# Both parts of a head's phi stacked in 128 rows for the product with the memory matrix

## The chip, the cores and the metric

The kernel runs as one program on one core of a Trainium2 chip. The metric is the device time of one execution in microseconds (us); lower is better.

## The reference

Four batches of eight heads (32 heads, 16 pairs of neighbouring heads), 576 tokens and 64 channels a head. Each head gets causal softmax attention and a second term, a read from a memory matrix; the two are mixed by a gate. Two MLP layers follow.

```python
scores = scale * q @ k.T                      # causal, then softmax -> a
local = a @ v
q_p = phi(q)                                  # phi(x) = where(x > 0, x, exp(x) - 1) + 1
mem_ret = einsum('bhsd,bhde->bhse', q_p, M_prev)          # M_prev: 64 x 64 for each head
mem_norm = einsum('bhsd,bhd->bhs', q_p, z_prev)[..., None] + 1e-06
mem_out = mem_ret / mem_norm
g = sigmoid(beta)
attn = g * mem_out + (1 - g) * local
x = attn as (B*S, H*D)
x = (sigmoid(x @ w_gate) * (x @ w_val)) @ w_out           # 2304 tokens, 512 -> 1536 -> 512
h = x @ w_in                                              # 512 -> 2048
out = (h * clip(h + 3, 0, 6) / 6) @ w_out2                # 2048 -> 512
```

## The kernel before

**Precision.** TensorE multiplies numbers rounded to fp32r. The kernel splits an operand x into a rounded part `hi` and a remainder `lo = x - hi` and adds several products. ScalarE (ACT) writes `hi` as it copies a block out of PSUM, VectorE (DVE) then writes `lo` with a subtraction that reads the same PSUM block and `hi`.

**The product with the memory matrix.** phi of a pair lies with tokens in the partitions; TensorE turns it (`turn_phi`, L859), so that a PSUM block has channels in the partitions: rows 0 to 63 belong to the even head of the pair, rows 64 to 127 to the odd one. Before, `move_hi` (L1140) rounds the block into `phit_hi` (128 rows, 576 columns) and `move_lo` (L1488) writes `phit_lo`. Each comes in two pieces: piece 0 has 512 columns and lies in bank TURN, piece 1 has 64 columns and shares a bank with a turned block of probabilities. The weights `m_hl[odd]` (128 x 128) hold head `odd`'s matrix in its own 64 rows alone, rounded in its own 64 columns, the remainder in the other 64; the rest of the tile is zero (a memset on GpSimd, L715). `times_mem` runs four matmuls a head: 128 columns with `phit_hi`, 128 with `phit_lo`, 448 with `phit_hi`, 448 with `phit_lo`, into `head_out` in banks AOUT and AOUT + 1. `times_v` adds the probabilities times v to the same place. Then ACT copies the 64 rows with the remainders' products to `x_low` (`x_lower`, L1198) and DVE adds them to the other 64 rows, into `x_new` (`x_sum`, L1544), which frees the banks (`x_done`).

**The order of work.** Each engine runs an instruction stream in a fixed order; semaphores tie the streams together. The first pairs (0 to 3) are prepared in a lead-in (`lead`) with fp32 data and don't use `m_hl`. Pairs 4 to 15 do. Pair 4's phi is turned and moved in the last step of the lead-in, that of pairs 5 to 15 in the steps of the main part. The main part is a sequence of steps `step(n, p, ...)`, with p = 0 and p = 1; two of them make a pair. In each, TensorE does, slot by slot (i = 0 to 4): scores of head (n, p), units of the first MLP (`FILL`: G and V are gate and value units, O output units), the products of the head of pair n - 1 (`times_mem`, `times_v`, in slot 0), and transposes of the probabilities of the head before (`turn_head`, L846). All products of the kernel have line L805 in the profile, since one helper `mm` issues them.

In a step with p = 1 slot 0 ends with `turn_phi(n, 0)`, which waits for `phi_ready`: DVE scales phi (`phi_scaled`, L1522) after the value unit V5 of the same slot. Slot 1 then begins with the scores and the output units O0 and O1, and ends with `turn_head(.., 0)`, which writes into bank AOUT + 1 and so waits for `x_done`. In the same slot ACT's order is: phi piece 0, the exponential of tile 1, `x_lower`, the rounding of the memory matrix (`high_m`, L1205), two weight blocks. DVE's is: phi piece 0, `x_sum`, two results Y (L1705 or L1707), and `low_q` (L1456), which writes the remainder of the next head's q from two SBUF tiles. The mask of the next score tile (L1540) is behind it; `scores` for tile i + 2 waits for the mask of tile i.

```python
elif i < 2:
    pe.wait_ge(x_done, 2 * n + odd)              # in turn_head
if j == 0:
    pe.wait_ge(phi_ready, n + 1)                 # in turn_phi
```

GpSimd splits k and v and writes the remainders of the weight blocks (`low_w`, L662). SyncE (SP) issues the loads; `load_m` is the last in a step with p = 1. After the last pair of a batch the attention output of that batch is cut into `x_hi` and `x_lo`, which gives ACT, DVE and GpSimd more work in that pair's last step. After some 577 us the attention is over; the rest is the MLPs.

Of the kernel before, what the change touches and what calls it, by code (L numbers as in the profile page):

```python
# [31 lines left out]
def attention_and_mlps(nc, qk_t, q_n, v_n, mem, z, beta, w_gate, w_val, w_out1, w_in, w_out2, out):  # L32
# [33 lines left out]
    def sb(name, shape, dt):  # L66
        size = 4
        for s in shape[1:]:
            size *= s
        at = top[0]  # L70
        top[0] += (size + 31) // 32 * 32
        assert top[0] <= nc.sbuf_usable_end, (name, top[0], nc.sbuf_usable_end)
        return nc.alloc_sbuf_tensor_at(name, shape, dt, offset=at)
# [51 lines left out]
    z_b = sb("z_b", [P, P], F32)  # L125
    m_st = sb("m_st", [P, D], F32)
    m_hl = [sb(f"m_hl{j}", [P, P], F32R) for j in two]
# [3 lines left out]
    znorm, znorm_e, zinv, zscale = [sb(x, [P, QT, 2], F32) for x in ("znorm", "znorm_e", "zinv", "zscale")]  # L131
    phit_hi = sb("phit_hi", [P, S], F32R)
    phit_lo = sb("phit_lo", [P, S], F32R)

# [60 lines left out]
    with ExitStack() as ctx:  # L195
# [9 lines left out]
        def other(odd):  # L205
            return own(1 - odd)
# [25 lines left out]
        ld_qk, ld_v, ld_phi, ld_m, ld_beta = [sem(x) for x in ("ld_qk", "ld_v", "ld_phi", "ld_m", "ld_beta")]  # L232
        init, m_zero, v_zero = sem("init"), sem("m_zero"), sem("v_zero")
        g_e, g_1, g_r, gates = sem("g_e"), sem("g_1"), sem("g_r"), sem("gates")
# [182 lines left out]
        def _(sp):  # L417
# [32 lines left out]
            def load_m(n):  # L450
                sp.dma_start(m_st[:, :], mem[bass.ds(n, 1), :, :].rearrange("a r c -> (a r) c")).then_inc(ld_m, DMA)

# [155 lines left out]
        def _(pool):  # L608

            for s, c in ((w_done, NST), (f_gout, 1), (f_vout, 1), (f_val, 1), (f_out, 1), (f_y, OU),  # L610
                         (hi_done, PIECES * FIRST), (lo_done, PIECES * FIRST), (ld_qk, 2 * DMA * (FIRST + 1)),
                         (ld_v, 2 * DMA * FIRST), (v_hi_done, 2 * FIRST), (v_ready, 2 * FIRST),
                         (ld_m, DMA * FIRST), (m_hi_done, 2 * FIRST), (m_ready, 2 * FIRST), (xc_hi, DT),
                         (xc_lo, DT - len(MIDDLE_X)), (xc_lo_mid, len(MIDDLE_X))):
                pool.sem_inc(s, c)
# [80 lines left out]
            def lead(n, p):  # L696
                u, turn = 2 * n + p, n >= 1 or p == 1

                def block():
                    k = first_block(n, p)  # L700
                    if k is not None:
                        low_w(0, k)

                cut_k(n + p, 1 - p)
                if p == 0:
                    if turn:
                        scaled_by_rows(u, 1)
                    phi_by_z(n)
                    block()
                else:  # L710
                    block()
                    scaled_by_rows(u, 0)
                if (n, p) == (0, 0):
                    for j in two:
                        pool.memset(m_hl[j][:, :].bitcast(F32), 0.0).then_inc(m_zero, 1)  # L715
                if n == FIRST and p == 1:
                    cut_v(n, 0)
# [83 lines left out]
        def _(pe):  # L801
# [60 lines left out]
            def times_mem(n, odd):  # L862
                pe.wait_ge(m_ready, 2 * (n + 1))
                pe.wait_ge(lo_done, piece_phi(n, 1) + 1)
                pe.wait_ge(x_done, 2 * n + odd)
                for a, b in ((0, P), (P, S)):
                    mm(head_out(a, b), m_hl[odd][:, :], phit_hi[:, a:b], True, False)
                    last = mm(head_out(a, b), m_hl[odd][:, :], phit_lo[:, a:b], False, False)
                last.then_inc(mem_done, 1)
# [237 lines left out]
        def _(act):  # L1107
# [15 lines left out]
            def move_hi(n, p, kind, i, r):  # L1123
                nn = n if p else n - 1
                if kind == "phi":
                    if i == 0:
                        act.wait_ge(mem_done, 2 * n)
                    act.wait_ge(turned, piece_phi(n, i) + 1)
                    dst, src = (phit_hi[:, 0:(QT - 1) * P], ps[:, TURN, 0:(QT - 1) * P]) if i == 0 else \
                        (phit_hi[:, (QT - 1) * P:S], ps[:, turn_bank(r, 0), 2 * P - TAIL:2 * P])  # L1130
                else:
# [68 lines left out]
            def high_m(n):  # L1200
                if known(n, 1):
                    act.wait_ge(mem_done, 2 * n)
                act.wait_ge(ld_m, DMA * (n + 1))
                for j in two:
                    act.activation(m_hl[j][own(j), own(j)], m_st[own(j), :], ACT.Copy).then_inc(m_hi_done, 1)  # L1205

# [4 lines left out]
            def lead(n, p):  # L1211
# [38 lines left out]
                else:  # L1250
# [12 lines left out]
                    move_hi(n, p, "head", 3, None)  # L1263
                    act.wait_ge(m_zero, 2)
                    high_m(n)
# [185 lines left out]
        def _(dve):  # L1451
# [21 lines left out]
            def move_lo(n, p, kind, i, r):  # L1473
                nn = n if p else n - 1
                if kind == "phi":
                    dve.wait_ge(hi_done, piece_phi(n, i) + 1)
                    cols = slice(0, (QT - 1) * P) if i == 0 else slice((QT - 1) * P, S)
                    src = ps[:, TURN, 0:(QT - 1) * P] if i == 0 else ps[:, turn_bank(r, 0), 2 * P - TAIL:2 * P]
                    dst, hi = phit_lo[:, cols], phit_hi[:, cols]
                else:  # L1480
# [44 lines left out]
            def low_m(n):  # L1525
                dve.wait_ge(m_hi_done, 2 * (n + 1))
                for j in two:
                    dve.tensor_tensor(m_hl[j][own(j), other(j)], m_st[own(j), :], m_hl[j][own(j), own(j)].bitcast(F32), ALU.subtract).then_inc(m_ready, 1)  # L1528

# [281 lines left out]
```

## Time and profile before

| | us |
|---|---|
| median of 3 runs | 1085.59 |
| range of the runs | 1085.3 to 1085.91 |
| the profiled execution | 1083.96 |
| its span, first to last instruction | 1082.1 |
| TensorE matmul busy in it | 1058.4 (98%) |
| DVE busy | 700.5 (65%) |
| ACT busy | 629.2 (58%) |
| GpSimd (POOL) busy | 546.4 (50%) |

The granted TensorE clock was full speed in the whole span. Busy times are unions over the span. Matmuls are pipelined: their durations overlap, so what one costs is read from the distance between starts.

### The profile page before, as it was taken

The page shows a single profiled execution, that of the slowest core. Times are in us where ns is not written, and L with a number is a line of the kernel's source. Part 1 is how long each engine was busy: PE and PEld are TensorE (multiplying, and loading weights), DVE is VectorE, ACT ScalarE, POOL GpSimd, SP SyncE. Part 2 cuts the span into 40 slices and gives each one's busy share as a digit, 9 for nine tenths or more (in the row PEclk, how much of TensorE's full clock was granted, in tenths as well). Part 3 has the DMA queues.
Part 4 walks back from the last instruction along what each step waited for, and adds up shares of the span by engine and source line. Part 5 has one row for each costly group of instructions (what it writes and reads, how often), then busy time and mean ns, then how long its engine had stood idle before and what let it go on. Part 6 is the DMA issues. An engine that isn't in the chain of part 4 may idle for free.

```text
span 1082.1 us, 20618 instructions
## 1 busy us (share of the span) xinstructions
PE 1058.4 (98%) x6784; PEld 991.2 (92%) x6784; DVE 700.5 (65%) x1521; ACT 629.2 (58%) x1414; POOL 546.4 (50%) x560
## 2 busy tenths in 40 slices
PE   5999999999999999999999999999999999999998
PEld 4778999999999999999999999989889888888897
DVE  5997766767767768766736444566577555665553
ACT  5787676677676776776754433455556343453333
POOL 5897567668657668766645654247880011000000
PEclk9999999999999999999999999999999999999999
DMA  8553343442542443443223335344545544454411
GB/s 191 137 134 86 101 108 84 125 108 70 131 114 67 119 112 86 106 116 97 61 69 109 87 99 175 118 166 146 191 162 163 152 122 117 118 175 117 119 58 58
DMA packets 124620, 126.50 MB, mean 117 GB/s; under 512 B 10352, under 2 KB 90736, under 8 KB 124272
## 3 DMA queue, kind: packets, MB, share of 16 engines
q1 hardware_dynamic: 124240, 121.67, 40.6%
q10 hardware_dynamic: 288, 3.67, 0.9%
q8 instruction: 50, 0.82, 0.3%
q14 instruction: 42, 0.34, 0.1%
HBM read 105.91 MB, written 19.40 MB: 116 GB/s over the span
## 4 chain that ended last, share of the span: by engine, by line
PE 91%; DVE 5%; issue 2%; ACT 1%; DMA 1%; SPq 0%; DVEq 0%; ACTq 0%
PE ps L805 86%; PE ps L846 4%; PE ps L859 1%; DVE q_s L1456 1%; DVE prob L1540 1%; DMA stage<-w_val 1%; DVE Y L1707 0%; DVE m_hl L1528 0%; DMA qk_st<-qk_t 0%; DVE pt_lo L1488 0%; DVE phi L1522 0%; DVE Cb L1732 0%; DVE x_lo L1555 0%; DVE znorm_e L1512 0%; ACT h_gate L1319 0%
## 5 line engine op out<-in xcount | busy, mean ns | idle before, releaser
L805 PE MATMUL ps<-x_hi,WG 128*128 128x288 f32 x1536 | 324.8, 297 | 1.6 <-DVE pt_lo L1488 1.5
L805 PEld LDWEIGHTS ps<-x_hi,WG 128*128 128x128 f32 x1536 | 251.4, 188 | 5.3 <-DVE h_val L1685 2.3
L805 PE MATMUL ps<-x_lo,WG 128*128 128x288 f32 x768 | 226.2, 295 | 0.0
L805 PE MATMUL ps<-XC,WC 128*128 128x384 f32 x1008 | 202.5, 336 | 2.1 <-DVE Cb L1732 1.7
L805 PEld LDWEIGHTS ps<-XC,WC 128*128 128x128 f32 x1008 | 180.2, 188 | 17.6 <-issue 3.2
L662 POOL TENSOR_TENSOR WG<-stage,WG 128x512 fp32r<-128x512 f32 x96 | 128.6, 1354 | 100.0 <-ACT WG L1168 100.0
L805 PE MATMUL ps<-wo,G_hi 128*128 128x512 f32 x540 | 168.0, 392 | 0.0
L805 PE MATMUL ps<-h_hi,WO 128*128 128x288 f32 x768 | 164.5, 297 | 0.2 <-DVE Y L1707 0.2
L690 POOL TENSOR_SCALAR prob<-prob,rscale 128x128 f32<-128x128 f32 (+4 forms) x160 | 110.8, 711 | 76.4 <-DVE rscale L1500 76.4
L805 PEld LDWEIGHTS ps<-x_lo,WG 128*128 128x128 f32 x768 | 144.3, 188 | 0.4
L1732 DVE TENSOR_TENSOR Cb<-ps,Cb 128x384 f32<-128x384 f32 x168 | 89.1, 554 | 83.3 <-PE ps L805 81.4
L805 PEld LDWEIGHTS ps<-h_hi,WO 128*128 128x128 f32 x768 | 126.2, 188 | 0.9 <-DVE Y L1707 0.4
L1185 ACT ACTIVATE prob<-prob,nmax 128x128 f32<-128x128 f32 (+4 forms) x160 | 95.9, 601 | 45.8 <-DVE nmax L1540 45.4
L805 PE MATMUL ps<-h_lo,WO 128*128 128x288 f32 x384 | 113.0, 294 | 0.0
L805 PEld LDWEIGHTS ps<-wo,G_hi 128*128 128x128 f32 x540 | 99.1, 188 | 10.8
L805 PE MATMUL ps<-wo,G_lo 128*128 128x512 f32 x270 | 107.2, 397 | 0.0
L1354 ACT ACTIVATE raw<-Cb 128x384 f32<-128x384 f32 x96 | 50.2, 523 | 78.5 <-DVE Cb L1732 76.8
L1540 DVE CUSTOM_DVE_ANT_0 prob<-ps,mask 128x128 f32<-128x128 f32 (+4 forms) x160 | 85.9, 538 | 9.6 <-PE ps L805 5.8
L1488 DVE TENSOR_TENSOR pt_lo<-ps,pt_hi 128x128 fp32r<-128x128 f32 (+4 forms) x120 | 58.5, 488 | 45.7 <-ACT pt_hi L1140 45.7
L805 PE MATMUL ps<-k_hi,q_s 128*128 128x128 f32 (+2 forms) x192 | 74.7, 395 | 10.9 <-DVE k_lo L1462 8.2
L1360 ACT ACTIVATE G_hi<-raw 128x384 fp32r<-128x384 f32 x96 | 50.5, 526 | 57.9 <-DVE raw L1736 57.7
L1685 DVE TENSOR_TENSOR h_val<-h_gate,ps 128x288 f32<-128x288 f32 x96 | 43.0, 448 | 61.9 <-PE ps L805 37.6
(137 smaller groups left out, 1983.5 us busy)
## 6 DMA issues: line engine op xcount, KB each, us to landing
WC<-w_in_parts SPq DMA_DIRECT2D x112, 256.0 KB, 2.7
stage<-w_out SPq DMA_DIRECT2D x64, 256.0 KB, 2.8
qk_st<-qk_t SPq DMA_DIRECT2D x54, 288.0 KB, 4.2
stage<-w_gate SPq DMA_DIRECT2D x48, 256.0 KB, 3.7
stage<-w_val SPq DMA_DIRECT2D x48, 256.0 KB, 3.2
w_in_parts<-WC SPq DMA_DIRECT2D x42, 256.0 KB, 2.1
qn_st<-q_n SPq DMA_DIRECT2D x16, 256.0 KB, 3.4
w_in_parts<-WC ACTq DMA_DIRECT2D x2, 1792.0 KB, 7.3
```

What stands on the lines that cost most here:

```text
L662: pool.tensor_tensor(lo, stage[k % NST][:, :], hi.bitcast(F32), ALU.subtract).then_inc(w_done, 1)
L690: pool.tensor_scalar(t, t, rscale[o][:, i:i + 1], 1.0, ALU.mult, ALU.mult).then_inc(normed, 1)
L805: return pe.matmul(o, l, r, start=start, stop=stop, skip_group_check=True)
L846: last = pe.transpose(ps[:, turn_bank(r, i), k * rows:k * rows + P], prob[odd][:, p_off[i] + k * P:p_off[i] + (k + 1) * P], ident[:, :])
L859: last = pe.transpose(ps[:, TURN if j == 0 else turn_bank(r, 0), o:o + P], phi[:, t, :], ident[:, :])
L1185: act.activation(dst, dst, ACT.Exp, scale=-1.0, bias=nmax[p][:, j:j + 1], accum_out=rsum[p][:, j:j + 1]).then_inc(exped, 1)
L1354: act.activation(raw[y % 2][:, :], Cb[y][:, :], ACT.Relu, bias=3.0).then_inc(c_relu, 1)
L1360: act.activation(G_hi[y][:, :], raw[y % 2][:, :], ACT.Copy, scale=1.0 / 6.0).then_inc(g_hi_done, 1)
L1488: dve.tensor_tensor(dst, src, hi.bitcast(F32), ALU.subtract).then_inc(lo_done, 1)
L1540: dve.tensor_tensor_reduce(dst, score(p, j), bias, -1.0, MOST, ALU.add, ALU.min, nmax[p][:, j:j + 1]).then_inc(maxed, 1)
L1685: dve.tensor_tensor(h_val[here], h_gate[here], ps[:, unit_bank(GV + g, alone), 0:HALF], ALU.mult).then_inc(f_vout, 1)
L1732: dve.tensor_tensor(Cb[y][:, :], prod_bank(s, i), Cb[y][:, :], ALU.add).then_inc(c_add, 1)
```

## The change

One tile `phit` of 128 rows, 2 heads and 576 columns takes the place of `phit_hi` and `phit_lo`. For each head the rounded phi stands in the head's own 64 rows and its remainder in the other 64, so one matmul over 128 rows multiplies both. The weights need the matrix in both halves of the rows: it is loaded twice and rounded in 128 rows.

```diff
-    m_st = sb("m_st", [P, D], F32)
+    m_st = sb("m_st", [P, 2, D], F32)
-    phit_hi = sb("phit_hi", [P, S], F32R)
-    phit_lo = sb("phit_lo", [P, S], F32R)
+    phit = sb("phit", [P, 2, S], F32R)
...
# load_m, SP
-                sp.dma_start(m_st[:, :], mem[bass.ds(n, 1), :, :].rearrange("a r c -> (a r) c")).then_inc(ld_m, DMA)
+                for half in two:
+                    sp.dma_start(m_st[own(half), :, :], mem[bass.ds(n, 1), :, :].rearrange("a (j r) c -> (a r) j c", j=2)).then_inc(ld_m, DMA)
...
# lead, POOL
-                if (n, p) == (0, 0):
-                    for j in two:
-                        pool.memset(m_hl[j][:, :].bitcast(F32), 0.0).then_inc(m_zero, 1)
...
# times_mem, PE
-                    mm(head_out(a, b), m_hl[odd][:, :], phit_hi[:, a:b], True, False)
-                    last = mm(head_out(a, b), m_hl[odd][:, :], phit_lo[:, a:b], False, False)
+                    last = mm(head_out(a, b), m_hl[odd][:, :], phit[:, odd, a:b], True, False)
...
# move_hi, ACT, kind "phi"
-                    dst, src = (phit_hi[:, 0:(QT - 1) * P], ps[:, TURN, 0:(QT - 1) * P]) if i == 0 else \
-                        (phit_hi[:, (QT - 1) * P:S], ps[:, turn_bank(r, 0), 2 * P - TAIL:2 * P])
+                    act.activation(phit[own(0), 0, cols], src[own(0), :], ACT.Copy)
+                    dst, src = phit[own(1), 1, cols], src[own(1), :]
...
# move_lo, DVE, kind "phi"
-                    dst, hi = phit_lo[:, cols], phit_hi[:, cols]
+                    dve.tensor_tensor(phit[other(0), 0, cols], src[own(0), :], phit[own(0), 0, cols].bitcast(F32), ALU.subtract)
+                    dst, src, hi = phit[other(1), 1, cols], src[own(1), :], phit[own(1), 1, cols]
...
# high_m, ACT, and low_m, DVE
-                    act.activation(m_hl[j][own(j), own(j)], m_st[own(j), :], ACT.Copy).then_inc(m_hi_done, 1)
+                    act.activation(m_hl[j][:, own(j)], m_st[:, j, :], ACT.Copy).then_inc(m_hi_done, 1)
-                    dve.tensor_tensor(m_hl[j][own(j), other(j)], m_st[own(j), :], m_hl[j][own(j), own(j)].bitcast(F32), ALU.subtract).then_inc(m_ready, 1)
+                    dve.tensor_tensor(m_hl[j][:, other(j)], m_st[:, j, :], m_hl[j][:, own(j)].bitcast(F32), ALU.subtract).then_inc(m_ready, 1)
```

## Rows read from the trace of the kernel before

**Rows 1.** The page: the chain that ended last, shares of the span by engine.
```profile
PE 91%; DVE 5%; issue 2%; ACT 1%; DMA 1%; SPq 0%; DVEq 0%; ACTq 0%
```

**Rows 2.** Timeline, 283 to 294 us, PE: start us, us, engine line, tiles.
```profile
283.79 0.23 PE L805 MATMUL ps<-phit_hi,m_hl 128*128 128x128 f32 x1
...
284.42 0.47 PE L805 MATMUL ps<-pt_hi,v_hl 128*128 128x128 f32 x2
...
286.11 0.65 PE L859 MATMUL ps<-ident,phi 128*128 128x128 f32 x4
...
289.20 0.29 PE L805 MATMUL ps<-h_hi,WO 128*128 128x288 f32 x1
...
289.51 0.30 PE L846 MATMUL ps<-ident,prob 128*128 128x128 f32 x1
...
292.74 0.38 PE L805 MATMUL ps<-k_hi,q_s 128*128 128x288 f32 x1
```

**Rows 3.** The same stretch, DVE, ACT and POOL; in brackets idle time and releaser.
```profile
285.21 0.81 DVE L1522 TENSOR_TENSOR phi<-phi,zscale 128x640 f32<-128x640 f32 x1
...
286.86 0.60 ACT L1140 ACTIVATE phit_hi<-ps 128x512 fp32r<-128x512 f32 x1 [0.91 <-PE ps L859]
...
287.35 0.50 ACT L1185 ACTIVATE prob<-prob,nmax 128x256 f32<-128x256 f32 x1
...
287.49 0.69 DVE L1488 TENSOR_TENSOR phit_lo<-ps,phit_hi 128x512 fp32r<-128x512 f32 x1 [0.34 <-ACT phit_hi L1140]
...
287.97 0.64 ACT L1198 ACTIVATE x_low<-ps 64x576 f32<-64x576 f32 x1
...
288.64 0.76 DVE L1544 TENSOR_TENSOR x_new<-ps,x_low 64x576 f32<-64x576 f32 x1 [0.46 <-ACT x_low L1198]
...
290.10 0.87 POOL L657 TENSOR_TENSOR v_hl<-v_st,v_hl 128x320 fp32r<-128x320 f32 x1
...
290.29 1.30 DVE L1456 SCALAR_TENSOR_TENSOR q_s<-qk_st,q_s 64x576 fp32r<-64x576 f32 x1
...
290.93 3.06 POOL L662 TENSOR_TENSOR WG<-stage,WG 128x512 fp32r<-128x512 f32 x2
...
292.22 0.62 ACT L1185 ACTIVATE prob<-prob,nmax 128x384 f32<-128x384 f32 x1 [1.59 <-DVE nmax L1540]
```

**Rows 4.** The same place in another pair, timeline at 203 to 206 us.
```profile
203.65 0.60 ACT L1140 ACTIVATE phit_hi<-ps 128x512 fp32r<-128x512 f32 x1 [0.83 <-PE ps L859]
...
205.54 0.76 DVE L1544 TENSOR_TENSOR x_new<-ps,x_low 64x576 f32 x1 [0.57 <-ACT x_low L1198]
```

**Rows 5.** Timeline, PE, at the ends of two pairs.
```profile
424.50 0.37 PE L805 MATMUL ps<-x_hi,WG 128*128 128x288 f32 x1 [0.46 <-DVE pt_lo L1488]
...
507.51 0.37 PE L805 MATMUL ps<-x_hi,WG 128*128 128x288 f32 x1 [0.32 <-DVE pt_lo L1488]
```

**Rows 6.** Timeline, DVE and PE, last step of the lead-in.
```profile
88.97 0.69 DVE L1488 TENSOR_TENSOR phit_lo<-ps,phit_hi 128x512 fp32r<-128x512 f32 x1 [0.23 <-ACT phit_hi L1140]
...
89.58 0.28 DVE L1488 TENSOR_TENSOR pt_lo<-ps,pt_hi 128x128 fp32r<-128x128 f32 x1
89.77 0.21 DVE L1488 TENSOR_TENSOR phit_lo<-ps,phit_hi 128x64 fp32r<-128x64 f32 x1
...
...
90.09 1.50 PE L846 MATMUL ps<-ident,prob 128*128 128x128 f32 x12 [0.71 <-issue]
```

**Rows 7.** Timeline, POOL and DVE, 15 to 18 us.
```profile
15.01 0.36 POOL L715 MEMSET m_hl<- 128x128 f32 x2
...
16.10 1.41 POOL L647 TENSOR_TENSOR k_lo<-qk_st,k_hi 128x576 fp32r<-128x576 f32 x1
...
16.38 1.16 DVE L1512 TENSOR_SCALAR znorm_e<-znorm 128x10 f32<-128x10 f32 x1
```

**Rows 8.** Timeline, SP, the load of the memory matrix and the next issue.
```profile
299.94 0.91 SPq L451 DMA_DIRECT2D m_st<-mem  x1
308.15 0.39 SPq L440 DMA_DIRECT2D v_st<-v_n  x1
```

More of the change, by code:

```diff
@@ L232, in attention_and_mlps @@
         ld_qk, ld_v, ld_phi, ld_m, ld_beta = [sem(x) for x in ("ld_qk", "ld_v", "ld_phi", "ld_m", "ld_beta")]
-        init, m_zero, v_zero = sem("init"), sem("m_zero"), sem("v_zero")
+        init, v_zero = sem("init"), sem("v_zero")
         g_e, g_1, g_r, gates = sem("g_e"), sem("g_1"), sem("g_r"), sem("gates")
@@ L612, in _ @@
                          (ld_v, 2 * DMA * FIRST), (v_hi_done, 2 * FIRST), (v_ready, 2 * FIRST),
-                         (ld_m, DMA * FIRST), (m_hi_done, 2 * FIRST), (m_ready, 2 * FIRST), (xc_hi, DT),
+                         (ld_m, 2 * DMA * FIRST), (m_hi_done, 2 * FIRST), (m_ready, 2 * FIRST), (xc_hi, DT),
                          (xc_lo, DT - len(MIDDLE_X)), (xc_lo_mid, len(MIDDLE_X))):
@@ L1128, in move_hi @@
                     act.wait_ge(turned, piece_phi(n, i) + 1)
-                    dst, src = (phit_hi[:, 0:(QT - 1) * P], ps[:, TURN, 0:(QT - 1) * P]) if i == 0 else \
-                        (phit_hi[:, (QT - 1) * P:S], ps[:, turn_bank(r, 0), 2 * P - TAIL:2 * P])
+                    cols = slice(0, (QT - 1) * P) if i == 0 else slice((QT - 1) * P, S)
+                    src = ps[:, TURN, 0:(QT - 1) * P] if i == 0 else ps[:, turn_bank(r, 0), 2 * P - TAIL:2 * P]
+                    act.activation(phit[own(0), 0, cols], src[own(0), :], ACT.Copy)
+                    dst, src = phit[own(1), 1, cols], src[own(1), :]
                 else:
@@ L1202, in high_m @@
                     act.wait_ge(mem_done, 2 * n)
-                act.wait_ge(ld_m, DMA * (n + 1))
+                act.wait_ge(ld_m, 2 * DMA * (n + 1))
                 for j in two:
-                    act.activation(m_hl[j][own(j), own(j)], m_st[own(j), :], ACT.Copy).then_inc(m_hi_done, 1)
+                    act.activation(m_hl[j][:, own(j)], m_st[:, j, :], ACT.Copy).then_inc(m_hi_done, 1)
             def x_high(n, p):
@@ L1263, in lead @@
                     move_hi(n, p, "head", 3, None)
-                    act.wait_ge(m_zero, 2)
                     high_m(n)
```

## The prediction

> **What bounds the kernel now.** I read the page first: matmuls are busy 98% of the span, and the chain that ended last lies on TensorE for 91% [rows 1]. So a matmul removed is time won, unless the engine then waits for something. Second, I read the timeline of one pair of the main part, first TensorE's rows alone, then the other engines'. What matters is not who is busy but at which instructions TensorE's program waits. Two pairs lie between 424.50 and 507.51, so one takes some 41.5 us [rows 5]; DVE and ACT are idle over a third of the span, yet around the moves of phi, in a step with p = 1, two waits are tight.
>
> The first is in front of the four transposes of phi. They start at 286.11, and DVE's scaling of phi ends at 285.21 + 0.81 = 286.02 [rows 2, 3]: the engine gets there just as its data is ready. The second is in front of the first transpose of probabilities. The output product before it starts at 289.20, a 288-column product holds the array some 0.13 us (0.20 for 448 columns would make it so, and the rows of output products stand at this distance), but the transpose starts only at 289.51, 0.11 after `x_new` has ended at 288.64 + 0.76 = 289.40. So TensorE already waits 0.18 us there for DVE, and the chain runs: transposes of phi, ACT `phit_hi`, ACT exponential, ACT `x_low`, DVE `x_new`, TensorE [rows 2, 3]. Whatever is put into this chain is paid in full. It is the place into which the change puts work.
>
> **What it takes from TensorE.** The four products of a head start at 283.79 and the next group at 284.42: 0.63 us, in which each shape occurs twice, so the removal of one of each saves 0.315 us [rows 2]. Twelve pairs have two heads, 24 x 0.315 = 7.6 us if all of it counted.
>
> It doesn't. The even head's products lie in the step with p = 0, where no tight wait follows: 12 x 0.315 = 3.8 us won. The odd head's lie in the step with p = 1, between the value unit V5 and the transposes of phi. Those wait for DVE's scaled phi, which depends on V5 and not on these products. TensorE comes 0.3 us earlier and waits 0.3 us longer: won is 0 (at most 0.02). That holds for 11 of the 12 odd heads, since in 11 steps (pairs 5 to 15) phi is turned; the last odd head has no such transposes behind it, 0.3 us. Sum: 4.1 us won.
>
> **What it adds to ACT and DVE.** Both moves of piece 0 become two instructions of 64 rows with 512 columns each. `x_low` with 64 rows and 576 columns takes 0.64 us, and the 128-row copy of 512 columns 0.60, so rows cost nothing and columns all [rows 3]: each half costs what the whole did. On ACT the next instruction starts 0.49 us after the move (286.86, 287.35), so `x_low` comes 0.49 later. On DVE the move lasts 0.69 and the next starts after 0.61 [rows 6]. Step by step from ACT's start H = 286.86: second half of the copy starts H + 0.49, ends H + 1.09; DVE's first half starts H + 1.12, its second H + 1.73, `x_new` can start at H + 2.35; `x_low` ends at H + 1.11 + 0.49 + 0.64 = H + 2.24, a little before. Before, `x_new` started at 288.64 = H + 1.78. So it is late by 0.57 us, and so is the transpose. In another pair, where `x_new` started at H + 1.89 [rows 4], it is late by 0.46. Of the 11 steps 7 are like the first pair and 4 like the second: 7 x 0.57 + 4 x 0.46 = 5.8 us lost. That no 64-row subtraction from PSUM into the other 64 rows is in the trace leaves its price open: between 0.2 us (were it to go at the pace of the 64-column piece) and 0.76 us (`x_new`, 64 rows, 576 columns); I take 0.69, the same columns.
>
> The Trainium skill says of this (VectorE: DVE Perf Modes, the errata section) that an instruction of VectorE costs a fixed part and its columns, whatever its rows; it speaks against the change. By its figures, 120 + 512 cycles at 0.96 GHz, a half is 0.66 us as an estimate, against 0.69 by the row: the loss would be some 0.05 us a step less.
>
> **What of that is given back.** At three pair ends TensorE waits for `pt_lo`: 0.46 us at 424.50, the like at the first batch's end, and 0.32 at 507.51 [rows 5]. What it waits for there hangs on GpSimd's work and a load, not on TensorE's own pace, so a TensorE that comes later waits less: 0.46 + 0.46 + 0.32 = 1.2 us back.
>
> Why doesn't DVE's delay reach further? Behind `x_new` come two results Y and then `q_s`, which takes 1.30 us. That is more than its 576 columns need (0.76 for `x_new`): it starts at 290.29, GpSimd's v remainder ends at 290.97, and 0.6 us later `q_s` is done. It waits for GpSimd to finish. Started 0.57 later, at 290.86, it still finds the same end at 290.97, so it ends at the same time and the mask behind it too [rows 3]. The extra 64-column halves (0.13 us each, 0.21 less the overlap of 0.08) fall on ACT into an idle of 1.59 us [rows 3, 6], on DVE in front of Y results that wait for TensorE. Uncovered they would cost 11 x 0.13 = 1.4 us.
>
> **The lead-in.** In its last step pair 4's phi is moved with nothing else to do: ACT `phit_hi`, then DVE `phit_lo` at 88.97 and the pieces behind it, for which 12 transposes of TensorE wait (0.71 us idle at 90.09) [rows 6]. Here ACT's 0.49, DVE's 0.61 and a second 64-column half of 0.13 add up: 1.2 us lost.
>
> **The memset.** The two zero fills of `m_hl` take 0.36 us at 15.01, in front of k's rounding and its remainder, 16.10 to 17.51. DVE's `znorm_e`, 10 columns, takes 1.16 us from 16.38: it ends as GpSimd's remainder ends, and phi's scaling and its transposes hang on it [rows 7]. All that comes 0.36 earlier: 0.36 us won, nothing if another wait takes its place.
>
> **Nothing.** `m_hl` keeps its instructions and their columns, in 128 rows instead of 64. `m_st` gets a second load: its issue is the last of the step, it takes up to 0.91 us of SP, and SP's next issue is 8 us later [rows 8]. Without that gap, it would delay weights by 0.9 us a pair.
>
> **The sum.** -4.1 + 5.8 - 1.2 + 1.2 - 0.4 = +1.3 us. The profiled execution took 1083.96, so 1085.3; it lay 1.6 under the median of 1085.59, which becomes 1086.9.
>
> **The rivals.**
> Rival 1, `q_s` misses GpSimd's gap. My start for it, 290.86, is only 0.11 us ahead of the end at 290.97. If it comes after the next weight block has begun (290.93, two in 3.06 us, so 1.53 each), it waits until 292.46 and ends at 293.1 instead of 291.59. The mask and its maximum, which came at 292.19 (the exponential waited 1.59 us for it), then come at some 293.7. TensorE's last scores need it; they began at 292.74 and with my delay begin at 293.3: 0.45 us more a step, 11 x 0.45 = 5, and at the two batch ends a DVE 1.5 us later may cost 1 each instead of giving back: 1086.9 + 5 + 3 = 1094, or 1091 if the ends hold. It decides once the halves on DVE cost over 0.11 us more than I take. For it: the small margin. Against it: 0.11 us is still a margin, and in pairs like rows 4 it is larger. The Trainium skill's page SBUF — State Buffer (who interferes with whom) states that a VectorE instruction with two SBUF inputs and a GpSimd instruction that reads SBUF exclude each other, and that the first holds on to its end. By that rule, which the 1.30 us bears out, a miss costs a whole GpSimd instruction, while the halves of phi, with one SBUF input, never wait.
>
> Rival 2, the saving arrives in full: the other engines absorb their work, as an idle of 35 to 42% suggests. Then 24 x 0.315 + 0.4 = 8 us, 1077.6. The two tight waits of rows 2 and 3 are against it.
>
> Rival 3, half of it: the halves run quicker than I take (towards 0.2 us), or TensorE's wait at the transposes is mostly its own latency. With a delay of 0.2 us a step instead of 0.53, of which three ends give back 0.6, and 0.7 in the lead-in, the sum is -4.1 + 2.2 - 0.6 + 0.7 - 0.4 = -2.2: 1083.4.
>
> Rival 4, nothing is given back and the small halves are uncovered: 1.2 + 1.4 more, 1089.5.
>
> **How the numbers follow.** My forecast 45%, 1086.9, its own range 1085 to 1088.5; rival 1 20%; rival 2 6%; rival 3 14%; rival 4 15%. A measurement of this kernel tells changes over 0.2%, 2.2 us, from none. Faster by that: rival 2 and half of rival 3 with what lies beside it, 14%. Slower, over 1087.8: rival 1, rival 4 and the upper end of mine, 41%. Within: 45%. The range from 1082 to 1092 leaves out rival 2 and the worst half of rival 1.
>
> **What the profile after would show.** Products with `m_hl` at two a head, and 0.31 us for them. Transposes of phi starting with DVE's phi, with a wait of some 0.3 us in the steps with p = 1. `x_new` starting 2.35 us after ACT's first copy of phi, and the transpose behind it waiting 0.6 to 0.75 us instead of 0.18. `q_s` ending with the same distance to GpSimd's v remainder; if it lasts over 2 us, rival 1 holds. Pairs some 0.2 us longer than before, and shorter waits at the three ends. I am wrong if the waits lie elsewhere, above all if TensorE's order hides a wait I have read as latency.

## The result and the profile after

The changed kernel takes 1097.0 us (median, 1096.07 to 1098.24), the kernel before 1085.75 beside it (1085.3 to 1087.89): 1.01 times as long, 95% interval 1.0082 to 1.0119. So it is 11.3 us slower. The prediction, 1086.9 with a range from 1082 to 1092, named the two waits and the rival that came true, and missed the size: the time lies outside its range, and above the 1094 of that rival too.

On the page of the profile after, the matmuls do what was said: there are 48 fewer, 6736 instead of 6784. But the chain that ended last lies on TensorE for 72% only, against 91% [rows 1], and TensorE's groups show where it stands idle. In front of the transposes of probabilities it was 2.3 us before:

```profile
PE 1056.4 (96%) x6736; PEld 986.9 (90%) x6736; DVE 716.1 (65%) x1545; ACT 639.2 (58%) x1438; POOL 546.4 (50%) x558
...
PE 72%; DVE 12%; ACT 9%; issue 6%; DMA 0%; DVEq 0%; ACTq 0%; SPq 0%
...
L843 PE MATMUL ps<-ident,prob 128*128 128x128 f32 x480 | 79.8, 282 | 13.2 <-issue 12.9
```

The timeline of the changed kernel at the place of [rows 2, 3], start, duration, instruction, and in brackets the idle time before it with its releaser. First TensorE:

```profile
291.58 0.48 PE L802 MATMUL ps<-phit,m_hl 128*128 128x128 f32 x2
291.89 0.48 PE L802 MATMUL ps<-pt_hi,v_hl 128*128 128x128 f32 x2
...
293.47 0.28 PE L802 MATMUL ps<-pt_lo,v_hl 128*128 128x64 f32 x1
...
293.88 0.66 PE L856 MATMUL ps<-ident,phi 128*128 128x128 f32 x4
...
296.98 0.29 PE L802 MATMUL ps<-h_hi,WO 128*128 128x288 f32 x1
...
298.16 0.30 PE L843 MATMUL ps<-ident,prob 128*128 128x128 f32 x1 [0.88 <-issue]
...
301.88 0.29 PE L802 MATMUL ps<-k_lo,q_s 128*128 128x288 f32 x1
...
302.49 0.40 PE L802 MATMUL ps<-h_hi,WO 128*128 128x288 f32 x1 [0.32 <-DVE Y L1703]
```

A head's products now take 0.31 us (291.58 to 291.89) instead of 0.63. Then three waits: phi's transposes start 0.41 after the last product, 0.3 more than a product needs; the first transpose of probabilities 1.18 after its forerunner, where 0.13 would do; and an output product 0.61 after the last scores, some 0.48 too late, where TensorE did not wait before. The other engines in the same stretch:

```profile
293.02 0.81 DVE L1520 TENSOR_TENSOR phi<-phi,zscale 128x640 f32<-128x640 f32 x1
...
294.64 0.59 ACT L1127 ACTIVATE phit<-ps 64x512 fp32r<-64x512 f32 x1 [0.89 <-PE ps L856]
...
295.24 0.60 ACT L1138 ACTIVATE phit<-ps 64x512 fp32r<-64x512 f32 x1
...
295.87 0.51 ACT L1183 ACTIVATE prob<-prob,nmax 128x256 f32<-128x256 f32 x1
295.87 0.68 DVE L1476 TENSOR_TENSOR phit<-ps,phit 64x512 fp32r<-64x512 f32 x1 [0.92 <-ACT phit L1138]
...
296.49 0.65 ACT L1196 ACTIVATE x_low<-ps 64x576 f32<-64x576 f32 x1
296.57 0.69 DVE L1486 TENSOR_TENSOR phit<-ps,phit 64x512 fp32r<-64x512 f32 x1
...
297.30 0.76 DVE L1542 TENSOR_TENSOR x_new<-ps,x_low 64x576 f32<-64x576 f32 x1
...
297.92 0.88 POOL L657 TENSOR_TENSOR v_hl<-v_st,v_hl 128x320 fp32r<-128x320 f32 x1
298.09 0.82 DVE L1703 COPY Y<-ps 128x288 f32<-128x288 f32 x2
...
298.75 3.06 POOL L662 TENSOR_TENSOR WG<-stage,WG 128x512 fp32r<-128x512 f32 x2
298.94 1.72 DVE L1453 SCALAR_TENSOR_TENSOR q_s<-qk_st,q_s 64x576 fp32r<-64x576 f32 x1
...
300.69 0.56 DVE L1538 CUSTOM_DVE_ANT_0 prob<-ps,mask 128x384 f32<-128x384 f32 x1
```

Read it by start distances. With H = 294.64, ACT's second half starts at H + 0.60 and not at H + 0.49; DVE's first half at H + 1.23, its second 0.70 later and not 0.61; `x_new`, 0.73 after that, at H + 2.66 against the forecast H + 2.35. Each half costs its full length and a little more, while the whole moves of [rows 3, 6] let the next instruction in 0.11 and 0.08 us before their end. And `q_s` starts at 298.94, after the weight block has begun at 298.75: it has missed the gap behind `v_hl` and lasts 1.72 us.

The sums over the main part, by kind of wait, are in this table. The main part is here the stretch from the first product with `m_hl` to the first one of the last head, so 23 of the 24 heads' products lie in it. A wait is the distance of two starts on TensorE less the short distance that the same pair of shapes has elsewhere in the traces; the columns on the right are experiments told below. The steps are 11, but `q_s` stands in 10 of them only: the last has none.

```
us, sums over the main part   before  after  halves  twice  x first  x first
                                             (e2)    (e3)   (e4)     before (e5)
transposes of probabilities    2.1    11.3   10.3     8.8    under 0.4 under 0.4
output product behind scores   0       5.1    3.4     0.8    2.1      0
transposes of phi              0.7     4.1    0.7     0.7    4.0      0.7
pair ends                      2.4     2.0    1.6     1.5    1.1      2.4
length of the main part      476.6   487.6  489.4   485.0  472.9    474.8
```

The main part is 11.0 us longer: 9.2 + 5.1 + 3.4 - 0.4 of waits, 0.9 beside them (the output product behind a wait holds the engine some 0.1 longer), less 23 x 0.315 = 7.2. The largest other part is the lead-in. From its last product with `m_first` to the first with `m_hl` it took 12.5 us (83.21 to 95.73) and now 15.1 (84.29 to 99.35). Its rows after, the counterpart of [rows 6]:

```profile
89.42 0.59 ACT L1127 ACTIVATE phit<-ps 64x512 fp32r<-64x512 f32 x1 [0.41 <-PE ps L856]
...
90.03 0.59 ACT L1138 ACTIVATE phit<-ps 64x512 fp32r<-64x512 f32 x1
...
90.66 0.69 DVE L1476 TENSOR_TENSOR phit<-ps,phit 64x512 fp32r<-64x512 f32 x1 [0.82 <-ACT phit L1138]
...
92.89 0.42 DVE L1486 TENSOR_TENSOR pt_lo<-ps,pt_hi 128x256 fp32r<-128x256 f32 x1
92.96 2.61 PE L843 MATMUL ps<-ident,prob 128*128 128x128 f32 x12 [2.49 <-issue]
```

The windows of both kernels, columns PE, PEld, DVE, ACT and POOL busy (x instructions), granted clock, DMA share, GB/s; before first:

```profile
93.00:96.60 3.60, 3.60 (x28) 3.57 (x28) 1.85 (x10) 3.32 (x10) 2.13 (x5) 1.00 0.26 61
```

```profile
90.00:93.00 3.00, 0.51 (x6) 0.40 (x5) 2.23 (x6) 2.88 (x9) 2.24 (x4) 1.00 0.80 196
93.00:96.60 3.60, 3.60 (x18) 3.45 (x19) 3.50 (x12) 2.69 (x10) 0.00 (x0) 0.53 0.53 109
```

TensorE is idle for 2.49 us instead of 0.71, and behind that idle the granted clock is 0.53, its lower level of 1.2 GHz for nearly the whole window (before, it is 1.00 in both windows): the 12 transposes take 2.61 us instead of the 1.50 of [rows 6].

### The profile page after: what moved, and what is told of

Its sections match the earlier page's. It is cut to its first block, busy times and chain, and to the rows that moved or that the text cites. A ratio compares the mean times of both kernels' runs of the same rounds, so it can differ in the third digit from the quotient of the medians.

```text
span 1096.4 us, 20584 instructions
## 1 busy us (share of the span) xinstructions
PE 1056.4 (96%) x6736; PEld 986.9 (90%) x6736; DVE 716.1 (65%) x1545; ACT 639.2 (58%) x1438; POOL 546.4 (50%) x558
## 4 chain that ended last, share of the span: by engine, by line
PE 72%; DVE 12%; ACT 9%; issue 6%; DMA 0%; DVEq 0%; ACTq 0%; SPq 0%
PE ps L802 68%; PE ps L843 3%; ACT h_gate L1316 2%; DVE q_s L1453 2%; DVE h_val L1683 2%; ACT L1183 1%; ACT pt_hi L1138 1%; DVE h_lo L1548 1%; DVE phi L1520 1%; ACT WG L1166 1%; ACT L1316 1%; PE ps L856 1%; DVE Y L1705 1%; ACT prob L1183 1%; DVE prob L1538 1%
## 5 line engine op out<-in xcount | busy, mean ns | idle before, releaser
L843 PE MATMUL ps<-ident,prob 128*128 128x128 f32 x480 | 79.8, 282 | 13.2 <-issue 12.9
```

The lines of the kernel that those rows point to most:

```text
L843: last = pe.transpose(ps[:, turn_bank(r, i), k * rows:k * rows + P], prob[odd][:, p_off[i] + k * P:p_off[i] + (k + 1) * P], ident[:, :])
```

## The experiments

```
label                        median   range             ratio to before, 95% interval
e1_fewer_matmuls             1080.82  1080.26-1081.48   0.9955 [0.9938, 0.9972]
e2_halves                    1099.36  1097.81-1101.16   1.0126 [1.0109, 1.0143]
e3_twice_128                 1095.04  1094.37-1096.71   1.0086 [1.0069, 1.0103]
e4_x_first                   1083.53  1082.03-1084.26   0.9978 [0.9968, 0.9987]
e5_x_first_before            1082.18  1081.39-1083.19   0.9968 [0.9957, 0.9979]
e6_phi_early                 1084.98  1083.25-1085.62   0.9996 [0.9986, 1.0006]
e7_more_order                1088.08  1085.73-1088.87   1.0019 [1.0009, 1.0029]
e8_matrix_only               1084.40  1083.31-1085.36   0.9994 [0.9984, 1.0003]
e9_whole_lead                1082.24  1081.13-1082.65   0.9967 [0.9956, 0.9979]
e10_split_lead               1083.30  1081.60-1084.43   0.9977 [0.9968, 0.9986]
e11_x_first_before_again     1083.31  1081.06-1083.88   0.9974 [0.9963, 0.9986]
e12_whole_lead_alone         1096.45  1095.99-1096.58   1.0099 [1.0084, 1.0114]
```

**One part at a time.** The saving alone: the kernel before without the remainder's two products a head, which its output therefore leaves out.

```diff
-                    mm(head_out(a, b), m_hl[odd][:, :], phit_hi[:, a:b], True, False)
-                    last = mm(head_out(a, b), m_hl[odd][:, :], phit_lo[:, a:b], False, False)
+                    last = mm(head_out(a, b), m_hl[odd][:, :], phit_hi[:, a:b], True, False)
```

> The kernel before with the two products with phit_lo left out of times_mem and nothing else changed; the products of phi's remainder with the memory matrix are missing from its output. Theory A (the odd head's saving is lost in the wait for the scaled phi): 12 x 0.315 + 0.3 = 4.1 us won, 1081.6, and the transposes of phi wait some 0.3 us more in the steps with p = 1 while they start as long after DVE's phi as before. Rival B (all products count): 7.6 us won, 1078.1.

Measured: 5.2 us less against the runs of before (3.0 to 6.7 by the interval), of which the traces' main parts show 3.8 (476.6 to 472.8); the last head's 0.3 comes behind them. The odd heads' share is lost in front of phi's transposes, where the wait has grown from 0.7 to 4.0 us over the 11 steps. The prediction's 4.1 holds.

Its cost alone: the kernel before, each move of phi cut into two instructions of 64 rows.

```diff
                     dst, src = (phit_hi[:, 0:(QT - 1) * P], ps[:, TURN, 0:(QT - 1) * P]) if i == 0 else \
                         (phit_hi[:, (QT - 1) * P:S], ps[:, turn_bank(r, 0), 2 * P - TAIL:2 * P])
+                    act.activation(dst[own(0), :], src[own(0), :], ACT.Copy)
+                    dst, src = dst[own(1), :], src[own(1), :]
...
                     dst, hi = phit_lo[:, cols], phit_hi[:, cols]
+                    dve.tensor_tensor(dst[own(0), :], src[own(0), :], hi[own(0), :].bitcast(F32), ALU.subtract)
+                    dst, src, hi = dst[own(1), :], src[own(1), :], hi[own(1), :]
```

> The kernel before with both moves of phi cut into two instructions of 64 rows each, same tiles, four products a head as before: the change's work on ACT and DVE without its gain on TensorE. Theory A (an instruction on other rows than the one before it starts only when that one has ended, so the chain to x_new is 0.31 us longer than forecast and q_s misses GpSimd's gap): x_new 2.66 us after ACT's first copy, q_s 1.7 us long, and all the loss of the changed kernel plus the matmuls' 4.1: 11.3 + 4.1, some 1101. Rival B (the loss comes from the second load, the wider memory matrix or the lead-in, not from the halves): under 1092.

Measured: 13.7 us more by the ratio, with the same waits as the changed kernel at two of its places. So the loss comes with the halves. But the parts don't add up to the whole: in the main part the halves cost 12.8 us (489.4 against 476.6) and the saving gives 3.8, which makes 9.0, and the changed kernel lost 11.0. The other 2.0 show at the same two places. `x_new` starts at H + 2.54 here in 7 of the 11 steps and at H + 2.64 in 4, in the changed kernel at H + 2.66 in all; and `q_s` is held up (1.77 to 1.80 us long) in 8 of 10 steps, there in all 10. In those 7 steps `x_new` starts 0.62 us after the second half on DVE (294.74, 295.36), in the changed kernel 0.73. DVE's halves here write the rows that they read; in the changed kernel they write the other 64.

The same number of instructions and columns without the cut: each move of 128 rows done twice, the first time into a spare tile.

```diff
+                    act.activation(spare[0][:, slice(0, (QT - 1) * P) if i == 0 else slice((QT - 1) * P, S)], src, ACT.Copy)
...
+                    dve.tensor_tensor(spare[1][:, cols], src, hi.bitcast(F32), ALU.subtract)
```

> The kernel before with each move of phi done twice over all 128 rows, the first time into a spare tile: as many instructions and columns on ACT and DVE as in the halves, but all on 128 rows. Theory A (only a change of rows forbids the overlap): second copy 0.49 us after the first, x_new 2.35 us after the first copy as was forecast, q_s in time for GpSimd's gap and 1.3 us long or less, loss 5.8 + 1.2 - 1.2: some 1091.5. Rival B (two instructions from the same PSUM block never overlap, whatever their rows): as the halves, some 1101.

Measured: 9.3 us more by the ratio, 4.3 less than with the halves. The timeline of this kernel at the same place:

```profile
292.74 0.60 ACT L1132 ACTIVATE spare<-ps 128x512 fp32r<-128x512 f32 x1 [0.91 <-PE ps L860]
293.23 0.59 ACT L1142 ACTIVATE phit_hi<-ps 128x512 fp32r<-128x512 f32 x1
293.86 0.69 DVE L1482 TENSOR_TENSOR spare<-ps,phit_hi 128x512 fp32r<-128x512 f32 x1 [0.83 <-ACT phit_hi L1142]
294.47 0.68 DVE L1491 TENSOR_TENSOR phit_lo<-ps,phit_hi 128x512 fp32r<-128x512 f32 x1
295.18 0.76 DVE L1547 TENSOR_TENSOR x_new<-ps,x_low 64x576 f32<-64x576 f32 x1
```

Behind a 128-row move the next 128-row move starts 0.49 us later on ACT and 0.61 on DVE, as forecast from [rows 3, 6]; behind a 64-row half the other half starts 0.60 and 0.69 or 0.70 later. The durations are the same. `x_new` starts 0.71 us behind the last move and not 0.62, so it stands at H + 2.44 and not at the forecast H + 2.35, but earlier than with the halves. That is enough for `q_s` to come in time (0.76 us long) in 6 of 10 steps, against 2 with the halves; in the one shown it starts at 296.82, as the weight block does, and lasts 1.89.

Its matrix edits alone: the kernel before with the matrix in both halves, two loads and no zero fill, so that its products take in the other head's rows too.

> The kernel before with the changes to the matrix alone: two loads, m_st and m_hl filled in 128 rows, no zero fill; phi's moves and the four products as before, so its output mixes the two heads' phi. Theory A (these edits cost nothing): 1085.5 to 1086.2, less 0.4 if the zero fill's place in the lead-in counts. Rival B (the second load delays the weights): over 1088.

Measured: no difference (by the interval, from 1.7 us less to 0.3 more). The main part takes 476.6 us, the lead-in 12.5. The matrix edits cost nothing that can be seen; of the zero fill's 0.36 us nothing can be seen, since the start of these kernels scatters more (the last product with `m_first` starts anywhere from 83.05 to 84.39 over all the traces).

**Take the moves off the path.** If the loss is the wait for `x_new`, then `x_low` and `x_new` ahead of phi's moves take it away. In the changed kernel (e4) and in the one before (e5, and again as e11):

```diff
                 for i in range(QT):
+                    if (p, i) == (1, 1) and old:
+                        x_lower(n, p)
...
-                    if i == 1 and old:
+                    if i == 1 and old and p == 0:
                         x_lower(n, p)
```

and so with `x_sum` on DVE.

> The changed kernel with x_lower and x_sum put ahead of the moves of phi in slot 1 of the steps with p = 1, where ACT and DVE wait for the transposes of phi. Theory A (the loss is the moves' place in the chain to x_done): the wait of 1.05 us before the first transpose of probabilities is gone, q_s comes in time again; against the kernel before -4.1 for the matmuls, -1.9 for the wait of 0.18 that it had in 11 steps, +1.5 in the lead-in: some 1081. Rival B (DVE has too much work in this slot wherever it stands, the wait moves to the Y results or the next scores): over 1088.

> The kernel before (four products a head, phit_hi and phit_lo) with x_lower and x_sum ahead of the moves of phi, as in the last run. Theory A (the order frees the wait of 0.18 to 0.23 us that stood in front of the first transpose of probabilities in 11 steps): 2 us won, 1084. Then the change itself is worth, in this order, only 0.5 us (1083.5 against 1084), the gain of its products less its lead-in. Rival B (the order alone gives all of the 2.5 us and more): 1082 or less, the change gives nothing in either order.

Measured: 13.5 us less for the changed kernel, 2.4 under the kernel before. The wait at the first transpose is gone:

```profile
287.82 0.64 ACT L1196 ACTIVATE x_low<-ps 64x576 f32<-64x576 f32 x1
287.89 0.66 PE L856 MATMUL ps<-ident,phi 128*128 128x128 f32 x4
...
288.64 0.59 ACT L1127 ACTIVATE phit<-ps 64x512 fp32r<-64x512 f32 x1 [0.18 <-PE ps L856]
...
288.99 0.76 DVE L1544 TENSOR_TENSOR x_new<-ps,x_low 64x576 f32<-64x576 f32 x1
...
290.99 0.30 PE L802 MATMUL ps<-h_hi,WO 128*128 128x288 f32 x1
291.12 0.27 PE L843 MATMUL ps<-ident,prob 128*128 128x128 f32 x1
```

The transpose follows its forerunner after 0.13 us, and `x_low` lies in an idle of ACT that was there anyway, while TensorE turns phi. But the kernel before gains 3.5 us from the same order and is not slower than the changed one. By the traces the change then wins 1.9 us in the main part (474.8 to 472.9) and loses 2.6 in the lead-in (12.53 to 15.16). The expectation of e5 had been that the order would give little without the halves; it gave more. Its trace shows 1.8 us, about the 0.18 a step of [rows 2]; the other 1.7 of the medians stand in no trace (the profiled execution of the kernel before was 1.8 under its median, that of e5 1.0 over its own), and the second run (e11, 2.8 by the ratio) had 0.7 of them less.

**Try for the rest.** In e4 there are still 4.0 us of waits at phi's transposes and 2.1 at the output product. e6 also scales phi ahead of the multiplication of V5; e7 also moves the 64-column remainder behind two results Y and, in the lead-in, `x_high` and `x_rest` ahead of phi.

```diff
+                            if g == GV - 2 and scoring:
+                                phi_scaled(n)
                             if g == GV - 1:
-                                if scoring:
-                                    phi_scaled(n)
                                 hidden_lo(r, g)
```

> The changed kernel with x_lower and x_sum ahead of the moves, and DVE's scaling of phi put ahead of the value unit V5's product instead of behind it. Theory A (the odd head's saving is lost in the wait for the scaled phi): the transposes of phi no longer wait 0.22 to 0.45 us and 11 x 0.3 = 3.3 us come back, some 1080. Rival B (V5's product, 0.8 us later, is what the output units then wait for): 1083.5 or more.

> The kernel of the run before, and besides DVE's move of phi's 64-column piece behind the results Y of slot 2, and in the lead-in x_high and x_rest ahead of the moves of phi. Theory A: the wait of 0.2 us behind the last scores in 11 steps goes (2 us), and of the lead-in's 2.6 us wait 0.6 go, and with it perhaps the stretch of half TensorE clock behind it (1 to 1.7 us): some 1077. Rival B (each of these waits is followed by another of the same length): 1080 as the run before.

Both were misses: 1.5 and 4.6 us slower than e4. In e6 the wait at phi's transposes is gone and the one at the output product has grown from 2.1 to 9.4 us. The row:

```profile
289.76 0.64 ACT L1196 ACTIVATE x_low<-ps 64x576 f32<-64x576 f32 x1
...
292.36 0.69 DVE L1488 TENSOR_TENSOR phit<-ps,phit 64x512 fp32r<-64x512 f32 x1
...
293.08 0.82 DVE L1707 COPY Y<-ps 128x288 f32<-128x288 f32 x2
...
293.60 0.40 PE L802 MATMUL ps<-h_hi,WO 128*128 128x288 f32 x1 [0.67 <-DVE Y L1707]
```

V5's product is later, and with it what ACT does between it and `x_low`; so `x_low`, `x_new`, phi's four halves and Y are later, and TensorE needs Y's bank. What is taken from one wait comes back at the next. That DVE has no slack left in these steps is how I read it; no run isolates it. e7 adds a wait at the ends of two batches (0.88 us idle at 258.72, on Y), and its lead-in stays at 15.2 us: with `x_high` and `x_rest` ahead, the idle in front of the 12 transposes is 2.77 us.

**The lead-in.** e9 is e4 with pair 4's phi moved whole by one 128-row instruction on each engine, its products four to a head, each from its own 64 rows; e12 is the changed kernel with this alone.

```diff
+                    if isinstance(n, int) and n == FIRST:
+                        mm(head_out(a, b), m_hl[odd][own(odd), :], phit_w[0][own(odd), a:b], True, False)
+                        last = mm(head_out(a, b), m_hl[odd][own(odd), :], phit_w[1][own(odd), a:b], False, False)
...
```

> The changed kernel with x_low and x_new ahead of phi's moves in the steps, and in the lead-in pair 4's phi moved as before the change: all 128 rows by one instruction on each engine, its products four to a head, each from its own 64 rows. Theory A (the lead-in's 2.5 us came from the moves cut in halves, through the wait before the 12 transposes and the half clock behind it): last m_first product to first m_hl product 12.5 to 12.7 us instead of 15.2, the granted clock full throughout, first to last memory product about 472.9 plus four matmuls of 0.3, time 1082.2, against 1083.5 with the lead-in's moves in halves. Theory B (the lead-in lost through something else of the change, the m_hl moves for one): still 14.5 or more, and 1083.5 to 1084.5.

> The changed kernel in its own order, only the lead-in's phi of pair 4 moved whole, its products four to a head. Theory A: the lead-in gives its 2.5 back, less four matmuls of 0.3 which lie beside a wait that is there anyway; first to last memory product stays 487.6 or up to 1 more, time 1094.5 (1094.0 to 1095.3). Theory B (the lead-in's loss is made up later or has another cause): 1096.5 or more.

Measured: the lead-in takes 12.6 us in both, as before the change (12.5), and its clock is full. The counterparts of the rows after, from e9:

```profile
93.00:96.60 3.60, 3.60 (x27) 3.43 (x27) 2.25 (x11) 3.10 (x9) 1.81 (x4) 1.00 0.51 110
```

```profile
88.89 0.60 ACT L1146 ACTIVATE phit_w<-ps 128x512 fp32r<-128x512 f32 x1 [0.40 <-PE ps L857]
...
90.65 1.51 PE L844 MATMUL ps<-ident,prob 128*128 128x128 f32 x12 [0.71 <-issue]
```

So the halves cause all of the lead-in's 2.5 us. Part of it is paid back: the first pair is 1.1 us longer (42.20 against 41.07), 0.5 a head, since the four products from 64 rows hold TensorE for 0.82 us where two took 0.31:

```profile
96.38 0.90 PE L803 MATMUL ps<-phit_w,m_hl 64*128 64x128 f32 x4
97.20 0.59 PE L803 MATMUL ps<-pt_hi,v_hl 128*128 128x128 f32 x2
```

The medians move by 1.3 (e9 against e4), as expected, and by 0.6 (e12 against the changed kernel), where 2.5 had been expected: I had taken this price to lie beside a wait that is there anyway. By the traces less is left in both: the main part of e12 takes 489.1 us, 1.5 more, so that 0.9 remain, and that of e9 takes 474.8, 1.8 more than e4's, so that 0.7 remain and the 1.3 of the medians are in part luck.

e10 keeps the halves: a semaphore lets DVE start the first remainder as soon as its own half is moved, and the last mask goes ahead of `x_rest`.

> The changed kernel with x_low and x_new ahead of phi's moves in the steps; in the lead-in VectorE begins with the first half's remainder as soon as that half is moved (a semaphore of its own), and the mask of the last block is ahead of x_rest. Theory A: VectorE's chain sets the lead-in, so it begins 0.6 earlier and the mask 0.76 earlier: last m_first to first m_hl product 13.8 to 14.3 instead of 15.2, time 1082.3 to 1082.8. If the engine before the transposes still waits over 2 us the half clock stays and half of it is lost again. Theory B (something else sets the lead-in): 15 or more, 1083.5.

> The kernel before with x_low and x_new ahead of phi's moves, a second time, beside the changed kernel in the same order on the same chip: 1082.2 as in its first run (1081.4 to 1083.2). If the change pays in a good order, the one with the lead-in's phi moved whole is 0.5 or more faster than this; if not, they are within 0.5.

Measured, in the profiled execution: lead-in 13.8 us, the idle before the 12 transposes 1.89 instead of 2.45, and no half clock behind it; the transposes take 1.63 us. But e3 has the same idle, and its clock fell:

```profile
91.16 1.63 PE L844 MATMUL ps<-ident,prob 128*128 128x128 f32 x12 [1.89 <-issue]
```

```profile
92.19 2.09 PE L847 MATMUL ps<-ident,prob 128*128 128x128 f32 x12 [1.89 <-issue]
93.00:96.60 3.60, 3.60 (x18) 3.35 (x17) 3.44 (x13) 3.14 (x10) 0.04 (x1) 0.53 0.51 107
```

The first is e10, the other two e3. Nor was this execution like its fellows: it is the shortest of e10's 11. The traces of the changed kernel and of e4, which have one stretch of half clock, show a mean granted clock of 0.998, and 8 of e10's 11 runs show 0.998 too. So the shorter idle has not been shown to keep the clock; the median moves 0.2, within what such runs scatter. What the half clock costs can be read from the two traces: with the same idle, e3's lead-in takes 14.56 us and e10's 13.83, 0.7 less.

The kernels with x first against each other: 1082.24 for e9, and 1082.18 and 1083.31 for the two runs of the kernel before in the new order. The intervals cover each other. In the new order both kernels beat the kernel before, by 2.4 to 3.5 us; that the change adds to what the order gives is not shown.

## Why the prediction was wrong

**The matmuls' term, -4.1: right.** The trace of e1 shows 3.8 in the main part and 0.3 behind it. The argument that the odd heads' saving ends in front of phi's transposes holds at its place, 3.3 us over 11 steps.

**The term +5.8 for the wait for `x_new`: right place, wrong size.** It is 9.2 us. The step that failed reads "On ACT the next instruction starts 0.49 us after the move", and the same of 0.61 on DVE: I carried the overlap of two 128-row instructions over to 64-row halves. It does not hold there, which makes 0.11 + 0.09 + 0.11 = 0.31 us: `x_new` at H + 2.66 instead of H + 2.35. The first two, between the halves on ACT and on DVE, are shown by e2 against e3. The third, between the last move and `x_new`, is there in e3 as well (0.71 us) and gone in 7 steps of e2 (0.62), so it isn't a matter of halves alone. Duration by columns alone was right, 0.68 to 0.69, the other half's rows included, whose price the range had left open. (The Trainium skill's rule, VectorE: DVE Perf Modes, errata section, a fixed part and the columns whatever the rows, agrees; the estimate by it was 0.66.) Beyond the 0.31 no more is needed: 0.53 + 0.31 = 0.84 a step, times 11, is 9.2.

**`q_s`, forecast at nothing: rival 1.** Its condition was "once the halves on DVE cost over 0.11 us more than I take". `x_new` and `q_s` behind it came 0.31 later than I took, and in the stretch shown `q_s` missed GpSimd's gap by 0.19 us (298.94 against 298.75). Its mechanism is seen: 1.69 to 1.79 us long in all 10 steps, the mask behind it late. The sign given for it, over 2 us, was too strict: I took 1.53 us for each weight block, half of the 3.06 for two, but the one that `q_s` waits for takes 1.29, and the longer one of 1.81 is the one that meets a working `q_s`. Its price was forecast at 0.45 a step, 5 in all, at the last scores; it is 0.51 in 10 steps, 5.1, paid one place later, so that the good size is partly luck. The scores wait hardly at all, the results Y stand on DVE behind the mask, and the output product waits for their bank. I gave this 20% though the margin was a third of the error that it had to bear. The Trainium skill's page SBUF — State Buffer (who interferes with whom) has the rule that a VectorE instruction with two SBUF inputs and a GpSimd instruction that reads SBUF exclude each other; the 1.72 us against 0.76 agrees, and so do phi's halves, one SBUF input each, which take 0.68 to 0.69 us in all 24 cases beside a working GpSimd.

**Given back, -1.2: hardly.** At 507.51 the wait is gone, but at the two batch ends TensorE waits longer, for Y (0.59 us idle at 262.77 and 433.44, where it was some 0.46 [rows 5]). The pair-end waits sum to 2.0 us against 2.4. Rival 4 had this half.

**The lead-in, +1.2: it was 2.5.** DVE's first move starts 1.24 us after ACT's (89.42, 90.66) instead of 0.64, because it waits for both halves of ACT; that, the second half on DVE and the small ones delay the transposes by 1.8 us. The other 0.7 is the size of the half clock behind the long idle, as e3 against e10 has it. The prediction did not think of the clock.

**The memset, -0.4, and the matrix edits, nothing:** e8 shows no cost for the second load and the 128-row forms; the gain can't be told from the scatter of the start.

By these the sum is -3.8 (the saving of 23 heads less the wait at phi, 3.4 - 7.2) + 9.2 + 5.1 + 0.9 - 0.4 + 2.5 = 13.5 us of the 14.3 between the two profiled spans (1082.1, 1096.4). Of the rest, 1.1 lies before the last product with `m_first`, in work that the change does not touch but for the fill, and which scatters by as much between traces; 0.3 less is the last head's saving.

The medians differ by 11.3 and not by 14.3, since the profiled execution of the kernel before was 1.8 under its median and that of the changed kernel 1.2 over. The four runs of the changed kernel fall into two pairs: 1096.07 and 1096.15 with a mean granted clock of 1.000, 1097.85 and 1098.24 with 0.998, the profiled one among them. So half of its runs seem to have had no such stretch of half clock, and are still some 10.4 us slower than the kernel before. What stays open is why two runs of one kernel differ in this, and how much of the 1.9 us between the pairs is the clock's, which cost 0.7 in the traces.

## What to carry to other kernels

Price an instruction that is cut in two by the start distance of such halves, not by that of the whole instructions in the trace; if the trace has none, the end of one plus the start delay of an instruction that waits for nothing (here up to 0.04 us) is the bound that the range has to reach. Here the trace of before had such a pair: the four rows of the last section. Where a forecast rests on a gap that is met by a tenth of a microsecond, sum the errors of the chain ahead of it before giving the miss its chance. And look first whether the chain needs to pass through the moved work: here the place of one instruction on each of two queues was worth more than the change, with it or without.

## What the runs showed of the hardware

The overlap of neighbours depends on the rows that the two work on. On ACT a 128-row copy of 512 columns lets the next 128-row instruction start 0.11 us before its end and on DVE 0.08; between halves on rows 0 to 63 and 64 to 127 there is none, the second starts 0.01 to 0.02 us after the first has ended, in all 12 pairs of the changed kernel and of e2. The same shows in `m_hl`: two copies of 64 columns take 0.40 us in 128 rows each, and 0.54 in 64 rows each on different halves.

It isn't the number of rows. The trace of before has one instruction, `x_hi`, on either half, each time with 128 rows behind it. The first row here works on rows 0 to 63, the third on rows 64 to 127:

```profile
80.96 0.64 ACT L1209 ACTIVATE x_hi<-ps 64x576 fp32r<-64x576 f32 x1 [1.59 <-PE ps L805]
81.51 0.71 ACT L1185 ACTIVATE prob<-prob,nmax 128x512 f32<-128x512 f32 x1
...
89.52 0.65 ACT L1209 ACTIVATE x_hi<-ps 64x576 fp32r<-64x576 f32 x1
90.19 0.72 ACT L1185 ACTIVATE prob<-prob,nmax 128x512 f32<-128x512 f32 x1
```

Behind rows 0 to 63 the next starts 0.09 us before the end, behind rows 64 to 127 it starts 0.02 after it, and so at all four places of either kind. The other way round, on ACT the copy of phi's last 64 columns, rows 0 to 63, starts 0.10 us before the end of the 128-row copy ahead of it (298.66 + 0.28, 298.84), and in e2 the DVE half on rows 0 to 63 starts 0.08 to 0.09 before the end of a 128-row move, while in the changed kernel, where it writes rows 64 to 127, it starts 0.03 after it. `x_new` of these steps, rows 64 to 127, doesn't overlap a 128-row move (e3: 294.47 + 0.68, then 295.18), and starts 0.08 before the end of e2's half on rows 64 to 127 in 7 of 11 steps. All these rows fit one reading: two neighbours overlap when both begin at the same row, in what they read and in what they write. The other 4 steps of e2 don't fit it, and no run was made to test it.

What an idle of TensorE does to the clock is not settled by its length. Idles of 2.36 to 2.77 us in front of the 12 transposes of the lead-in went with a stretch of half clock (the changed kernel, e2, e4, e6, e7), idles of 0.67 to 0.71 did not (before, e1, e5, e8, e9, e11, e12), and of two idles of 1.89 us one did (e3) and one did not (e10). Four products from 64 rows held the array for 0.82 us, where the four from 128 rows of [rows 2] took 0.63.
